# Local attention with a gated expert: later tap sums, halved first softmax, one exp for three chunks, and more of chunk 0's sums on TensorE

## What is computed

```python
w = softmax(weight_gen, axis=-1)                    # [B, S, H, K], with 1e-9 added to the sum
x_unf = x_pad[:, idx, :].reshape(B, S, K, H, D // H)  # the K last tokens of each token, zeros ahead of a batch
attn = einsum('bshk,bskhg->bshg', w, x_unf)          # [B, S, D]
h = maximum(attn @ w_in, 0)                          # [B, S, F]
conv_out = sum over 3 taps of conv_w[k] * shifted h  # along S, per channel
gate = 1 / (1 + exp(-conv_out))
out = (h * gate) @ w_out                             # [B, S, D]
```

## Time and profile before

| | us |
|---|---|
| median of 3 runs (lowest, highest) | 716.75 (716.65, 717.0) |
| the profiled execution | 717.6 |
| its span, first to last record | 715.8 |
| TensorE busy | 704.5 (98%) |
| VectorE busy | 614.4 (86%) |
| GpSimd busy | 614.0 (86%) |
| ScalarE busy | 497.7 (70%) |

### The profile page before, as it was taken

How to read it: one execution, slowest core, us unless ns; L and a number is a source line. 1 busy time by engine, 2 the same in 40 slices (tenths; PEclk the granted TensorE clock), 3 DMA queues, 4 the chain that set the end, 5 groups by cost and what they waited for, 6 DMA issues and landing times.

```text
span 715.8 us, 9877 instructions
## 1 busy us (share of the span) xinstructions
PE 704.5 (98%) x3843; PEld 631.6 (88%) x3843; DVE 614.4 (86%) x551; ACT 497.7 (70%) x638; POOL 614.0 (86%) x285
## 2 busy tenths in 40 slices
PE   8997999999999999999999999999999999999998
PEld 8656899999999989998989898989999999999997
DVE  7999999999988899898898989898999989885630
ACT  2759877796767676776977676777777867676641
POOL 5999999999997999999899999989898899925310
PEclk9999999999999999999999999999999999999999
DMA  8320412002031222212030211203020200000001
GB/s 251 134 103 1 100 51 85 32 16 100 18 100 30 74 58 64 78 35 95 23 101 16 72 47 32 84 23 108 27 93 23 51 23 18 22 18 23 23 30 33
DMA packets 26297, 41.44 MB, mean 58 GB/s; under 512 B 3864, under 2 KB 23678, under 8 KB 24461
## 3 DMA queue, kind: packets, MB, share of 16 engines
q1 hardware_dynamic: 26250, 40.81, 18.6%
HBM read 28.02 MB, written 12.78 MB: 57 GB/s over the span
## 4 chain that ended last, share of the span: by engine, by line
PE 92%; DVE 3%; ACT 2%; DMA 1%; issue 1%; SPq 0%; ACTq 0%; DVEq 0%
PE out_ps L955 45%; PE z L933 40%; PE turn_ps L982 3%; PE turn_ps L955 2%; DMA x_win<-in_x 1%; DVE attn_a L814 1%; PE z L945 1%; DVE z L773 1%; DVE z L779 0%; PE z L993 0%; DVE attn_b L814 0%; ACT hidden L634 0%; PE z L955 0%; ACT gated L653 0%; DVE xb L824 0%
## 5 line engine op out<-in xcount | busy, mean ns | idle before, releaser
L486 POOL TENSOR_TENSOR weighted<-x_win,soft 128x1344 f32<-128x1344 f32 (+1 forms) x128 | 350.9, 2763 | 7.9 <-DMA x_win<-in_x 7.8
L955 PE MATMUL out_ps<-wo,gated 128*128 128x192 f32 x2000 | 346.0, 326 | 0.2
L955 PEld LDWEIGHTS out_ps<-wo,gated 128*128 128x128 f32 x2000 | 326.9, 190 | 8.2 <-ACT out_sb L689 0.7
L603 POOL TENSOR_TENSOR gated<-gated,hidden 128x1022 f32<-128x1022 f32 (+1 forms) x117 | 248.8, 2126 | 72.9 <-ACT gated L653 72.5
L773 DVE SCALAR_TENSOR_TENSOR z<-hidden,cw,z 128x1022 f32<-128x1022 f32 (+1 forms) x134 | 164.6, 1229 | 60.1 <-ACT z L640 59.3
L634 ACT ACTIVATE hidden<-z 128x1024 f32<-128x1024 f32 (+1 forms) x136 | 134.5, 989 | 108.3 <-PE z L933 99.4
L779 DVE SCALAR_TENSOR_TENSOR z<-hidden,cw,z 128x1022 f32<-128x1022 f32 (+1 forms) x134 | 166.2, 1240 | 4.2
L640 ACT ACTIVATE z<-hidden,cw 128x1022 f32<-128x1022 f32 (+1 forms) x134 | 144.9, 1081 | 4.2
L814 DVE TENSOR_REDUCE attn_a<-weighted 128x256 f32<-128x1792 f32 (+1 forms) x62 | 124.8, 2012 | 0.0
L653 ACT ACTIVATE gated<-z 128x1022 f32<-128x1022 f32 (+1 forms) x117 | 115.1, 984 | 10.5 <-PE out_ps L955 7.0
L933 PE MATMUL z<-xa_hi,wa_hi 128*128 128x512 f32 (+1 forms) x264 | 100.1, 458 | 5.8 <-ACT gated L653 5.2
(11 more groups left out here) (89 smaller groups left out, 389.6 us busy)
## 6 DMA issues: line engine op xcount, KB each, us to landing
x_win<-in_x SPq DMA_DIRECT2D x11, 1344.0 KB, 6.6
out<-out_sb SPq DMA_DIRECT2D x111, 96.0 KB
logits<-in_weight_gen SPq DMA_DIRECT2D x12, 224.0 KB
x_win<-in_x SPq DMA_DIRECT2D x2, 1008.0 KB
out<-out_sb SPq DMA_DIRECT2D x16, 84.0 KB
x_win<-in_x SPq DMA_DIRECT2D x1, 1176.0 KB
x_win<-in_x SPq DMA_DIRECT2D x1, 768.0 KB, 10.5
wo<-in_moe_w_out SPq DMA_DIRECT2D x1, 768.0 KB, 13.3
```

The lines of the kernel that those rows point to most:

```text
L486: return engine.tensor_tensor(to, rows, s, ALU.mult)
L603: nc.gpsimd.tensor_tensor(gated_flat(c, n), gated_flat(c, n), hidden[:, n % 3, 1:1 + c.size], ALU.mult) \
L955: last = nc.tensor.matmul(bank[0:end - begin, 0:D], gated[:, j, begin:end], wo[:, j, :], start=(j == 0), stop=(j == J - 1))
```

## The change

Five things are changed, all in the opening of the program.

1. *Softmax of chunk 0 in halves.* VectorE's one `normalise` of chunk 0 becomes two instructions of four tokens each; ScalarE copies each half by itself, the second into another PSUM bank (`soft_own_late`). Products of tokens 0 to 3 wait for the first half alone.
2. *More of chunk 0's sums on TensorE.* VectorE's sums of tokens 0, 2, 4 and 6 cover 128 channels, no longer 192. `sum_and_turn_last` is now also called for i = 0 and i = 4 and adds the last 64 channels of tokens 0 and 2, 4 and 6 out of GpSimd's products, whose taps lie innermost. Since TensorE now reads places of the ring, GpSimd's products 2 and 4 of chunk 1 wait for turning rounds 2 and 4.
3. *Later tap sums of chunk 1.* The sums of index 3 and up stand one step later, behind the convolution taps of that step.
4. *One exp for chunks 2, 3 and 4.* The group (3, 4) is gone; chunks 2 to 4 are one group, whose exp stands at k = 0, behind the relu of step 1. The maxima of chunks 3 and 4 stand ahead of all steps on VectorE, the subtractions on GpSimd behind products 3 and 4 of chunk 1 (`SHIFT_AT`).
5. *Logits of chunks 3 and 4* are loaded behind w_out, ahead of chunk 2's x.

The diff, without the declaration of the new semaphore:

```diff
@@ -14,6 +14,7 @@
 TOKENS = 8
 AHEAD = 2
 RING = 6
+SUM_LATER = 3
 OUTS = 4
 SLOTS = 8
 EARLY = 5
@@ -27,8 +28,9 @@
 BY_TENSOR = (1, 3, 5, 7)
 SUMS_FIRST = (0, 2, 4, 6)
 FIRST_ROWS = 8
-GROUPS = [(0,), (1,), (2,), (3, 4), (5, 6, 7, 8, 9), (10, 11, 12, 13, 14), (15, 16)]
+GROUPS = [(0,), (1,), (2, 3, 4), (5, 6, 7, 8, 9), (10, 11, 12, 13, 14), (15, 16)]
 GROUP_SLOTS = 5
+SHIFT_AT = {3: 3, 4: 4}
 EXPONENT = 6
 EXPONENTS = {}
 APART = 4
@@ -389,6 +392,7 @@
         attn_first = gated[0:FIRST.parts, len(BY_VECTOR), 0:TOKENS * D].rearrange("p (i d) -> p i d", d=D)
         soft_bank = z[2][:, 1, :]
         soft_own = soft_bank[0:FIRST.parts, 0:FIRST.tokens * HK]
+        soft_own_late = z[0][0:FIRST.parts, 1, 0:FIRST.tokens * HK]
 
         def places(c, i, count):
 
@@ -558,6 +562,8 @@
                     load_mask(c)
             load_x(CHUNKS[1])
             sp.dma_start(wo[:, :, :], w_out.rearrange("(j p) d -> p j d", p=P)).then_inc(s_weights_out, 16)
+            for c in CHUNKS[3:5]:
+                load_logits(c)
             for k in range(FIRST_STEP, LAST_STEP + 1):
                 for c in CHUNKS[2:]:
                     if group_of(c) in GROUPS[3:] and k == top_at(c) - 6:
@@ -582,10 +588,16 @@
                                     base=0, pattern=[[-1, P]], channel_multiplier=1).then_inc(s_ident, 1)
 
             def product(c, i):
-                if i == 0:
+                if c is FIRST and i < c.half:
+                    pool.wait_ge(s_soft_half, 1)
+                elif c is FIRST or i == 0:
                     pool.wait_ge(s_soft, c.number + 1)
                 if i == 0 or c in CHUNKS[:2]:
                     wait_x(pool, c, i)
+                if c is CHUNKS[1] and i == 2:
+                    pool.wait_ge(s_turned, 2)
+                if c is CHUNKS[1] and i == 4:
+                    pool.wait_ge(s_turned, 4)
                 if c is not FIRST and i % 2 == 0 and place_of(c, i) >= RING - 1:
                     pool.wait_ge(s_attn, summed_before(place_of(c, i) + 2 - RING))
                 multiply(nc.gpsimd, c, i, soft).then_inc(s_weighted, 1)
@@ -594,7 +606,7 @@
 
                 pool.wait_ge(s_weighted, products_before(c, c.tokens))
                 if c is FIRST:
-                    pool.wait_ge(s_soft_own, 1)
+                    pool.wait_ge(s_soft_own, 2)
                 normalise(pool, nc.gpsimd, CHUNKS[c.number + 1])
 
             def apply_gate(n):
@@ -606,6 +618,10 @@
             def step(k):
                 for c, i in SUM_AT.get(k + AHEAD, []):
                     product(c, i)
+                    for d in CHUNKS[3:5]:
+                        if c is CHUNKS[1] and i == SHIFT_AT[d.number]:
+                            pool.wait_ge(s_top, d.number + 1)
+                            subtract_top(nc.gpsimd, d)
                     if i == TOKENS - 1 and c is not LAST:
                         normalise_next(c)
                 for c in CHUNKS[2:]:
@@ -654,8 +670,11 @@
 
             def copy_soft():
 
+                half = FIRST.half * HK
+                act.wait_ge(s_soft_half, 1)
+                nc.scalar.copy(soft_own[:, 0:half], soft[0:FIRST.parts, 0:half]).then_inc(s_soft_own, 1)
                 act.wait_ge(s_soft, 1)
-                nc.scalar.copy(soft_own, soft[0:FIRST.parts, 0:FIRST.tokens * HK]).then_inc(s_soft_own, 1)
+                nc.scalar.copy(soft_own_late[:, half:2 * half], soft[0:FIRST.parts, half:2 * half]).then_inc(s_soft_own, 1)
 
             def exponent(g):
                 f, l = CHUNKS[g[0]], CHUNKS[g[-1]]
@@ -729,6 +748,8 @@
                 for c, r in TAKE_AT.get(k + 0.5, []):
                     take_turned(c, r)
                 n = STEP_OF.get(k)
+                if k == 0:
+                    exponent(GROUPS[2])
                 if n is not None:
                     gate(n)
                 if tile is not None and not (soon and k + 1 in STEP_OF):
@@ -750,7 +771,6 @@
             take_turned(FIRST, 2)
             take_turned(FIRST, 3)
             take_rest(1, wb_lo)
-            exponent(GROUPS[2])
             for k in range(FIRST_STEP, LAST_STEP + 1):
                 step(k)
             for t in range(FIRST_LAST_TILE, len(TILES)):
@@ -784,10 +804,22 @@
                 dve.wait_ge(s_gate, n + 1)
                 nc.vector.tensor_tensor(gated_banks(c, n), shifted(c, n, 1), conv(c, n), ALU.mult).then_inc(s_gated, 1)
 
+            def normalise_first(part):
+
+                c = FIRST
+                tokens = slice(part * c.half, (part + 1) * c.half)
+                if part == 0:
+                    dve.wait_ge(s_inverse, 1)
+                e = expo[0:c.parts, 0, 0:c.tokens * H * SLOTS].rearrange("p (i h s) -> p i h s", i=c.tokens, s=SLOTS)[:, tokens, :, 0:K]
+                r = inverse[0:c.parts, 0, 0:c.tokens * H].rearrange("p (i h) -> p i h", i=c.tokens)[:, tokens, :].unsqueeze(3) \
+                    .to_broadcast([c.parts, c.half, H, K])
+                to = soft[0:c.parts, 0:c.tokens * HK].rearrange("p (i k h) -> p i h k", i=c.tokens, k=K)[:, tokens]
+                nc.vector.tensor_tensor(to, e, r, ALU.mult).then_inc(s_soft_half if part == 0 else s_soft, 1)
+
             def own_product(c, i):
-                dve.wait_ge(s_soft_own, 1)
+                dve.wait_ge(s_soft_own, 1 if i < c.half else 2)
                 wait_x(dve, c, i)
-                multiply(nc.vector, c, i, soft_own).then_inc(s_weighted_dve, 1)
+                multiply(nc.vector, c, i, soft_own if i < c.half else soft_own_late).then_inc(s_weighted_dve, 1)
 
             def sum_taps(c, i):
                 first = i - i % 2
@@ -796,7 +828,7 @@
                         dve.wait_ge(s_weighted_dve, BY_VECTOR.index(i) + 1)
                     else:
                         dve.wait_ge(s_weighted, products_before(c, i + 1))
-                    nc.vector.tensor_reduce(attn_first[:, i, :], places(c, i, 1)[:, 0].rearrange("p (d k) -> p d k", k=K),
+                    nc.vector.tensor_reduce(attn_first[:, i, 0:P], places(c, i, 1)[:, 0, 0:P * K].rearrange("p (d k) -> p d k", k=K),
                                             AX.X, ALU.add).then_inc(s_attn, 1)
                     return
                 if i % 2 == 0:
@@ -853,8 +885,12 @@
                     apply_gate(m)
                 if n is not None:
                     last_tap(n)
+                for c, i in SUM_AT.get(k - 1, []):
+                    if c is CHUNKS[1] and i >= SUM_LATER:
+                        sum_taps(c, i)
                 for c, i in SUM_AT.get(k, []):
-                    sum_taps(c, i)
+                    if c is not CHUNKS[1] or i < SUM_LATER:
+                        sum_taps(c, i)
                 for c, r in LOW_AT.get(k + 0.5, []):
                     low_part(c, r)
                 for c in CHUNKS[2:]:
@@ -872,7 +908,8 @@
                 c = FIRST
                 shift(c)
                 sums(c)
-                normalise(dve, nc.vector, c)
+                normalise_first(0)
+                normalise_first(1)
                 for i in BY_VECTOR[:2]:
                     own_product(c, i)
                 shift(CHUNKS[1])
@@ -891,6 +928,8 @@
                 subtract_top(nc.vector, CHUNKS[2])
 
             attention_first()
+            for c in CHUNKS[3:5]:
+                maxima(c)
             for k in range(FIRST_STEP, LAST_STEP + 1):
                 step(k)
 
@@ -974,10 +1013,9 @@
                             src = attn_a[0:c.parts, i, :] if kind == "a" else attn_b[0:c.parts, i * P:(i + 1) * P]
                         else:
                             src = attn_first[:, i, 0:P]
-                        if c is FIRST and kind == "b" and i not in BY_TENSOR:
-                            for u, rows in ((i, slice(0, D2)), (i + half, slice(D2, P))):
-                                last = nc.tensor.matmul(bank_of(c, r)[rows, at * c.parts:(at + 1) * c.parts], attn_first[:, u, P:D],
-                                                        ident[0:c.parts, 0:c.parts], start=True, stop=True)
+                        if c is FIRST and kind == "b":
+                            if i not in BY_TENSOR:
+                                last = sum_and_turn_last(i)
                         elif c is not FIRST or i not in BY_TENSOR:
                             last = nc.tensor.transpose(bank_of(c, r)[:, at * c.parts:(at + 1) * c.parts], src,
                                                        ident[0:c.parts, 0:c.parts])
@@ -995,17 +1033,24 @@
 
             def sum_and_turn_last(i):
 
-                c, at, first = FIRST, i % 4, BY_VECTOR.index(i)
-                assert BY_VECTOR[first + 1] == i + 2
-                pe.wait_ge(s_weighted_dve, first + 2)
+                c, at = FIRST, i % 4
+                if i in BY_VECTOR:
+                    pe.wait_ge(s_weighted_dve, BY_VECTOR.index(i + 2) + 1)
+                else:
+                    pe.wait_ge(s_weighted, products_before(c, i + 3))
                 bank = bank_of(c, i // 4 * 2 + 1)
```

(11 more changed lines are left out.)

1 line of the change is left out of this document (added).

## The result

| | before | with the change |
|---|---|---|
| median of 17 runs (lowest, highest), us | 717.0 (716.65, 717.54) | 718.33 (717.95, 719.27) |
| the profiled execution | 717.6 | 718.14 |
| its span | 715.8 | 716.4 |

The ratio of the changed kernel to the one before is 1.0018, with a 95% interval of 1.0011 to 1.0024: 1.3 us slower, at the upper edge of what I had called within 0.2%. The forecast was 0.4 us slower. Of all executions in this document two, one of e5 (1033 us) and one of the kernel before (799 us), ran in a slower state at a lower granted clock, and no ratio counts them.

A forecast was written before the change was run, and what follows sets the result against it. TensorE's work was taken to bound all after 73 us, so only the opening could change. Terms 2.62 - 0.43 + 0.3 - 0.49 - 0.65 - 0.95 gave +0.4 us, 717.1 us; the 8-in-10 range was 716.0 to 720.1.

The forecast's parts named there:

- the rival with the strided loads: Opening: TensorE's new weight loads, reading every 28 bytes, run at a lower rate; 718.8 to 720.1 us, chance 0.34.
- the mark that I had named for it: In the opening, the first product still starting at 9.2 us, behind the landing of x.
- In(1): TensorE's ten matmuls of step 1, in the opening: forecast 2.5 us later than their 30.48 us.
- the sums on TensorE: Two longer TensorE blocks between 21.6 and 27.8 us: 2.62 us added, 0.43 absorbed, VectorE's saving not coming back there.
- Later tap sums and maxima: VectorE's list in the opening: 0.49 us regained at in(3), and 0.65 us at in(9).
- in(3): TensorE's ten matmuls of step 3: forecast 2.0 us later, starting at 43.3 us with no wait.
- in(9): TensorE's ten matmuls of step 9: forecast 1.4 us later, at 67.6 us, behind step 6's sigmoid.
- the burst: One exp for chunks 2 to 4: ScalarE loses 3.5 us near 66 us, of which 0.95 counts at in(10).
- in(10): TensorE's ten matmuls of step 10, before at 72.89 us: forecast 0.4 us later, at 73.3, directly behind the filler.
- gate(0): ScalarE's sigmoid of step 0, in the opening: forecast not held up by the moved exp, with 1.8 us of room.
- Behind it TensorE hardly stops, so whatever moves that start moves the end by as much.: From in(10) to the end: TensorE, busy in all 595.00 us from 75 to 670 us, passes on any shift in full.
- The other rivals: Opening: the burst holds up gate(0), 719.1 us for 2 us, chance 0.05; TensorE's longer list is absorbed, 714.6, chance 0.08.

The follow-up runs named there:

- e5: The changed kernel with GpSimd's products of chunk 0 laid as (tap, channel), so that TensorE's new weight loads are contiguous: 718.12 us, ratio 1.0013.
- e2: The kernel before with only the sums of chunk 0's last 64 channels moved to TensorE: 719.74 us, ratio 1.0037.
- e1: The changed kernel with VectorE again summing all 192 channels of chunk 0's even tokens: 717.03 us, ratio 0.9998.
- e10: The changed kernel with VectorE summing all 192 channels again, no filler matmuls, and the first output tile's copy ahead of step 9's sigmoid: 716.42 us, ratio 0.9991.
- e11: As e10, with GpSimd doing step 1's last product before chunk 2's first product: 716.10 us, ratio 0.9986.
- e12: As e11, with VectorE instead of GpSimd doing the two subtractions for chunks 3 and 4: 723.06 us, ratio 1.0083.
- e14: As e12, with the maxima of chunks 3 and 4 written to PSUM instead of SBUF: 715.69 us, ratio 0.9981.
- e7: The changed kernel with the tap sums of chunk 1 at their old place: 719.33 us, ratio 1.0032.
- e6: The changed kernel with separate exps for chunk 2 and for chunks 3 and 4, their maxima, subtractions and logits at their old places: 720.07 us, ratio 1.0040.
- E3: The changed kernel with ScalarE's copy of the first output tile ahead of step 9's sigmoid: 717.57 us, ratio 1.0008.
- e4: The changed kernel without the 14 filler matmuls ahead of step 10: 718.28 us, ratio 1.0016.

## Why the prediction was right, and where it was wrong

The time, 718.33, lies in the range. The direction was right and the size was not: 1.3 us for 0.4, a little outside the forecast's own range of 716.3 to 718.0. The range reached so far up only for the rival with the strided loads, which came at a fraction of its price; that it also held the step that I had missed is luck. Step by step, from S:

- **Softmax in halves: nothing.** Right in its worth; the mark that I had named for it did not come. The two halves take 0.98 us for 0.96. The first product was to start at 9.2 still, behind x; it started at 8.17 without a wait, as the first part of x had landed by then, and it is the second product that stands for x, by 1.01 us. In the one execution of e2, whose copy is in one piece, the first product waited 0.60 us for ScalarE's copy (to 8.83) and the second 0.54 for x all the same. In(1) shows that nothing comes of it: 19.06 to 19.11 from S in e1, e10, e11, e12 and e14, which have the halves and not the sums on TensorE, and 19.07 before.
- **The sums on TensorE.** Mechanism right, one term mis-sized. In(1) is 2.98 us later (2.5 predicted), and e2 by itself gives 2.99. The two blocks cost 1.88 and 1.86 us start to start. My 1.75 - 0.44 for each stood for the contiguous block, which takes 1.68 start to start: 0.38 us too little, which e5 gives back as 0.36. That is the price that I had bounded by nothing and by the half rate. The wait for wb_lo is 0.33 (in(0) to in(1) takes 2.77 us for 2.44); 0.3 was predicted.
- **The rival with the strided loads** named the right mechanism and the wrong size. A load grew by 8 ns; I had said that it decides from 18 ns. The Trainium skill, "Advanced Engine Details and Errata", section "SBUF Cachelines", is right that there is a penalty; it gives no figure, and what was measured is 1.16 times, not the factor of two that I had read out of it; my VectorE row, with 1.55, didn't bear on TensorE either. The value that I took, from the same engine and shape, was the nearer one.
- **Later tap sums and maxima.** Right in size. From in(1) to in(3) the kernel gains 0.60 (0.49 predicted), and in(3) doesn't wait; from in(3) to in(9) 0.64 (0.65). But e2, without the later sums, gains the same 0.60: the wait of in(3) goes because TensorE itself is late. What the later sums do is to make room for the two maxima of the burst that now stand ahead on VectorE; with these and without the later sums in(3) is 0.86 us and the end 0.8 us later (e7). The 0.64 is the maximum of chunk 4, gone from behind xb, for e2 and e6 don't have this gain and e7 does.
- **The burst.** Right. From in(9) to in(10) 1.19 us are gained (0.95: a wait costs a little more than its idle time), in(10) stands directly behind the filler, gate(0) isn't held (38.88), no table load is left near 66. The sum to in(10) is 2.98 - 0.60 - 0.64 - 1.19 = 0.55, where I had 0.4. It came out so near because two misses offset each other: in(1) 0.5 us later than worked out, the gains behind it 0.34 larger. E6 gives the burst 1.8 us at in(10) and 1.5 at the end by the medians, 1.1 from S.
- **"Behind it TensorE hardly stops, so whatever moves that start moves the end by as much."** This step failed. I had read the busy time of TensorE from 75 us on, 595.00 of 595.00, as proof that nothing else could be late. With the change it is 594.59: one wait of 0.41 us, which costs 0.69 from in(11) to in(12). VectorE was 1.7 us late from S at step 6, had no idle time to make it good, and I had followed it only as far as gate(7). TensorE had made up all but 0.5 of its own lateness by in(11), and the copy behind gate(9) had 0.72 us of slack, less than the 1.2 between the two. The text had named idle time between in(10) and 670 us as what would show it wrong, and that is what came; but no rival had it, with a price. E3 and e4 show it from both sides.
- **The other rivals** didn't come: gate(0) isn't held, and the longer list of TensorE isn't absorbed.

Together: 0.4 predicted at in(10), 0.15 more by the misses that offset each other, 0.67 by the copy behind gate(9), 1.22 in all.

## What to carry over

A busy share of one engine in a stretch tells what bounds it now, not how much the others can be late; follow every engine that the change delays past the mark until its list has an idle gap. Where a moved instruction ends up on an engine that is never idle (GpSimd here), the gain of the rest can stop there: e11 shows it with the clock at 1.00, e1 and e10 with the clock's fall beside it. And compare single executions from the landing of the first data, not from their start.

## What the runs showed of the hardware

- A weight load of 64 columns with a step of 28 bytes took 62 ns, a contiguous one 54 (1.16 times). VectorE's sums over a step of 768 bytes took 1.69 us each, over contiguous data 1.00.
- A VectorE `tensor_tensor` of 448 elements beside GpSimd's products took 1.56 and 3.17 us with both operands in SBUF, and 0.57 with one in PSUM (e12, e14).
- The granted clock was 0.83 over 10 us in e14 (70 to 80 us) and in e1 and e10 (60 to 70), behind several waits of TensorE of up to 2.2 us each, and the same kernel had a mean granted clock of 0.998 in some executions and 1.000 in others (e14: 6 of 11, 1.0 us slower by the medians). In e11 5 of 11 had a mean of 0.998 and were not slower (715.86 against 716.66); that GpSimd was the bound there may be why, but no run shows it. What decides it stays open.
- The landing of x, read at the VectorE product that it releases, moved by 1.2 us over the 14 profiled executions, twice what the two profiles differed by.
